# A fused attention and two-MLP kernel: earlier weight rounding, identity transposes at the start, and the gated values' low halves on GpSimd

## The chip, the cores and the metric

The kernel runs on one NeuronCore of a Trainium2 chip. The metric is the device time of one execution in microseconds. The kernel before takes 1164.55 us in the median of 3 runs (1164.22 to 1164.59).

## The reference

Sparse-threshold attention over 4 batches, 8 heads, 576 tokens and a head dimension of 64, then two MLPs over the 2304 tokens (512 to 2048 to 512), all in float32:

```python
scores = scale * q @ k.T
thresh = max(scores, -1) - tau
scores = where(scores >= thresh, scores, -1e9)
attn = softmax(scores)            # sum + 1e-9
x = (attn @ v) as [2304, 512]
h = x @ w_in1;  g = h * sigmoid(1.702 * h);      x = g @ w_out1
h = x @ w_in2;  g = h * tanh(softplus(h));       out = g @ w_out2
```

## The kernel before, in words

**Split precision.** Most products are made of three matmuls on values that are split into a rounded high half and the remainder, the low half: high times low, low times high, high times high. ScalarE writes the high half with a copy to a rounded type (lines with `_hi`), and another engine subtracts it from the raw value to get the low half (`_lo`). The low half lies in the same memory as the raw value. Batch 0's first 16 query tiles (steps 0 to 15) do without the split: their scores, transposes and PV products are plain float32 matmuls.

**Steps.** Attention is cut into N = 144 steps. Each handles one tile of 128 query rows against all 576 keys. All engines run the same software pipeline over a step counter n, each with an order written out by hand. For a step n TensorE makes the scores (`pe_scores`, one step ahead), VectorE takes the row maximum (`dve_max`), GpSimd works out the threshold (`pool_row`), ScalarE takes the exponential (`act_exp`), VectorE masks and sums (`dve_mask`, `dve_inv`, one step later), GpSimd or ScalarE normalises (`pool_norm` for the first 16 steps, `act_norm` afterwards), and two steps later TensorE transposes the probabilities by five matmuls with the identity (`pe_turn`), ScalarE copies them out of PSUM (`act_p_hi`) and VectorE writes their low half (`dve_p_lo`, from step 16 on). After each group of two or three steps TensorE multiplies with v (`pe_pv`), and the result is copied to x. In the first 16 steps this happens at even n: `act_x_first` copies the 64 rows of x from PSUM, and after every second head `act_x_hi_first` rounds a quarter of the first chunk of x, of which `dve_x_lo_first` writes the low half at the next n.

**The first MLP beside attention.** The tokens are taken in 9 chunks of 256 columns. Its work is a list of pieces: "up" pieces (two tiles of hidden features, called a pair) and "down" pieces. Each piece is made of two halves of twelve matmuls. `HALVES_AT[n]` says which halves TensorE makes in step n; a table of `READY` steps says from when a chunk's x is there, and the halves are spread evenly between those steps. The first 108 pieces run beside attention; the others (`ALONE`) follow when attention is over. After an up piece ScalarE takes tanh (`act_tanh`), VectorE multiplies (`dve_gate`), ScalarE rounds (`act_g_hi`) and VectorE subtracts (`dve_g_lo`, last in its step). The first down half of a quarter waits for the low halves of its two pairs.

**The weights of the first MLP** come in 16 pieces of 512 KB, in the order `W_ORDER`. `W_SLOT` gives each the step at which ScalarE rounds it (`act_w_hi`). SyncE issues the load four steps before. The low half is made in two halves, in the same step and the next on GpSimd (`pool_w_lo`), and for the first `W_FIRST` weights one step later on VectorE (`dve_w_lo`).

**Then** the second MLP runs alone, bound by TensorE; the change does not touch it.

A slot list of the tables, as the code works them out before the change: chunk 0 is ready at step 19, chunk 1 at step 43, and the last of 56 pairs beside attention is taken in the last steps. Between the second half of an up pair and the down half that needs it are three steps or more.

Of the kernel before, what the change touches and what calls it, by code (L numbers as in the profile page):

```python
# [29 lines left out]
GROUPS = []  # L30
# [73 lines left out]
for c in range(CHUNKS):  # L104
# [5 lines left out]
    CHUNK_GROUP.append(need)  # L110
READY = [GROUPS[g][4] + (4 if c == 0 else 8) for c, g in enumerate(CHUNK_GROUP)]

# [41 lines left out]
def thresholded_attention_two_mlps(nc, qt, kt, vt, tau, w_in1, w_out1, w_in2, w_out2, out):  # L154
# [3 lines left out]
    with ExitStack() as ctx:  # L158
# [209 lines left out]
        W_ORDER = [0, 1, 2, 3, 8, 9, 4, 5, 10, 11, 6, 7, 12, 13, 14, 15]  # L368
        W_SLOT = dict(zip((9, 12, 14, 17, 19, 21, 23, 24, 26, 28, 30, 31, 33, 34, 36, 37), W_ORDER))

# [8 lines left out]

        W_FIRST = 4  # L380

# [72 lines left out]
        def pe_scores(pe, n):  # L454
# [16 lines left out]
            for half in range(2):  # L471
# [4 lines left out]
                for t, (hd, u, kk) in enumerate(todo):  # L476
                    mm = pe.matmul(ps_s[:, 2 * (n % 2) + half, 0:HS], q_st[u % 2][:, q_cols(hd, i)],  # L477
                                   kk[u % 2][:, cols], start=t == 0, stop=t == len(todo) - 1)
            mm.then_inc(s["qk_done"], 1)

        def pe_turn(pe, n, tiles=range(NJ)):
# [187 lines left out]
        def act_g_hi(act, pair):  # L669
            hi, _, raw = slot_of(pair)  # L670
            act.wait_ge(s["h_read"], pair + 1)
            act.copy(hi, raw).then_inc(s["g_hi_done"], 1)

        def dve_g_lo(dve, pair):
# [214 lines left out]
        def _(pe):  # L889
            pe.wait_ge(s["ident_ready"], 1)  # L890
            pe_scores(pe, 0)
            for n in range(N + 3):
                if n < FRONT + 2:
                    if n >= 2:
                        pe_turn(pe, n - 2)
                    pe_scores(pe, n + 1)
                    if n - 3 in GROUP_AT:
                        pe_pv(pe, GROUP_AT[n - 3])
                    continue
                halves = HALVES_AT[n]  # L900
# [39 lines left out]
        def ups_at(n):  # L940
            return ups(PIECES_AT[n]) if 0 <= n < N + 3 else []

        @block.scalar
        def _(act):
            for n in range(-1, N + 4):
                for pair in ups_at(n - 1):
                    act_tanh(act, pair)
                if n < FRONT + 3:
                    if 0 <= n - 1 and not normed_by_pool(n - 1):
                        act_norm(act, n - 1)  # L950
                    if n >= 0:
                        act_exp(act, n)
                    if n >= 2:
                        act_p_hi(act, n - 2)
                    if n - 3 in GROUP_AT:
                        act_x_first(act, GROUP_AT[n - 3])
                    if n in X_HI_FIRST:
                        act_x_hi_first(act, X_HI_FIRST[n])
                    for u in Q_SCALE.get(n, []):
                        act_q_scale(act, u)  # L960
# [52 lines left out]
        def _(dve):  # L1013
# [3 lines left out]
            for n in range(-1, N + 4):  # L1017
# [17 lines left out]
                if n - 1 in X_HI:  # L1035
                    dve_x_lo(dve, X_HI[n - 1])
                if n - 1 in X_HI_FIRST:
                    dve_x_lo_first(dve, X_HI_FIRST[n - 1])
                if FRONT <= n - 2 < N:
                    dve_p_lo(dve, n - 2)  # L1040
                for pair in ups_at(n - 2):
                    dve_g_lo(dve, pair)
            for pair in ups_at(N + 2):
                dve_g_lo(dve, pair)
            last = []
# [34 lines left out]
        def _(pool):  # L1080
# [3 lines left out]
                               base=0, pattern=[[-1, P]], channel_multiplier=1).then_inc(s["ident_ready"], 1)  # L1084
            for n in range(-1, N):
                if n >= 1 and normed_by_pool(n - 1):
                    pool_norm(pool, n - 1)
                if n >= 0:
                    pool_row(pool, n)
                for u in KQ_PREP.get(n, []):  # L1090
                    pool_k_lo(pool, u)
                for u in V_PREP.get(n, []):
                    pool_v_lo(pool, u)
                for half in range(2):
                    if n - half in W_SLOT and w_place(W_SLOT[n - half]) > W_FIRST:
                        pool_w_lo(pool, W_SLOT[n - half], half)

        def sp_k(sp, u):
# [27 lines left out]
        def _(sp):  # L1126
# [8 lines left out]
            for n in range(N + 4):  # L1135
# [5 lines left out]
                if n - 3 in GROUP_AT:  # L1141
                    g = GROUP_AT[n - 3]
                    u = GROUPS[g][3]
                    if LAST_GROUP[u] == g and u + 2 < len(USES):
                        sp_v(sp, u + 2)
                if n + 4 in W_SLOT:
                    w_load(sp, 0, W_SLOT[n + 4])
                for g in groups_summed(n):
# [69 lines left out]
```

## Time and profile before

| | before |
|---|---|
| median of 3 runs | 1164.55 us |
| the profiled execution, its own time | 1164.05 us |
| its span, first to last instruction | 1162.3 us |
| mean granted TensorE clock | 0.995 |
| attention stage (last transposes of probabilities) | up to 647 us |

In the rows below PE is TensorE's matmul stream, PEld its weight loads, DVE VectorE, ACT ScalarE, POOL GpSimd, SPq SyncE's queue. A row of a timeline gives the start, the duration, the engine, the line of the code, output and inputs and the number of instructions merged; in brackets stands how long the engine had been idle and what released it. A group's row gives its busy time and the mean of one in ns, then the idle time before it.

### The profile page before, as it was taken

What the parts mean: (1) busy time and instruction counts of PE and PEld (TensorE: products, weight loads), DVE (VectorE), ACT (ScalarE), POOL (GpSimd) and SP (SyncE); (2) the same over time, 40 slices, a digit from 0 to 9 for tenths busy, and PEclk for the clock granted to TensorE, in tenths of its full rate; (3) what the DMA queues carried; (4) which work ended last, traced back from release to release, by engine and by line L of the source; (5) the groups of instructions that cost most, each with busy time, mean ns of one, the idle gap of its engine ahead of it and who ended that gap; (6) DMA issues with size and microseconds to landing.
All of it is one profiled execution on the core that took longest, in us unless ns stands there. A gap on an engine that the chain in (4) does not pass through costs nothing.

```text
span 1162.3 us, 19359 instructions
## 1 busy us (share of the span) xinstructions
PE 1118.1 (96%) x7472; PEld 1035.4 (89%) x7472; DVE 759.1 (65%) x1359; ACT 724.1 (62%) x995; POOL 295.4 (25%) x502
## 2 busy tenths in 40 slices
PE   8978889999999999999999999999999999999998
PEld 4568889998999999999999999998999989899997
DVE  4678788888888888888888434665433444344343
ACT  3678787767777777777767322467545554554453
POOL 3557674434444433344333000000000000000000
PEclk9989999999999999999999999999999999999999
DMA  2443534232143222233231003520010000000000
GB/s 65 140 131 114 158 86 111 59 94 85 48 111 91 64 82 77 79 105 83 70 103 28 26 19 106 190 76 28 6 49 1 28 28 28 28 28 28 1 28 27
DMA packets 92923, 78.71 MB, mean 68 GB/s; under 512 B 47520, under 2 KB 78752, under 8 KB 92832
## 3 DMA queue, kind: packets, MB, share of 16 engines
q1 hardware_dynamic: 92832, 77.49, 22.9%
q8 instruction: 59, 0.97, 0.4%
q14 instruction: 32, 0.26, 0.1%
HBM read 63.83 MB, written 13.63 MB: 67 GB/s over the span
## 4 chain that ended last, share of the span: by engine, by line
PE 78%; DVE 11%; ACT 7%; issue 3%; POOL 0%; DMA 0%; SPq 0%; ACTq 0%; DVEq 0%
PE ps_s L743 17%; PE ps_r L628 14%; PE ps_r L648 11%; PE ps_r L766 9%; PE ps_t L492 6%; PE ps_t L513 5%; PE ps_t L766 4%; PE ps_s L477 4%; PE ps_t L648 3%; PE ps_r L513 2%; PE ps_s L466 2%; DVE x_pair L585 2%; DVE pt_lo L574 2%; ACT pv_half_sb L544 1%; DVE neg_max L554 1%
## 5 line engine op out<-in xcount | busy, mean ns | idle before, releaser
L628 PE MATMUL ps_r<-x_hi,wi_lo 128*128 128x256 f32 x544 | 158.5, 291 | 2.7 <-DVE x_lo L701 2.7
L810 DVE COPY hidden<-ps_s 128x768 f32<-128x768 f32 x48 | 45.8, 956 | 170.5 <-PE ps_s L743 170.5
L628 PE MATMUL ps_r<-x_lo,wi_hi 128*128 128x256 f32 x544 | 154.2, 284 | 0.0
L628 PE MATMUL ps_r<-x_hi,wi_hi 128*128 128x256 f32 x544 | 154.2, 283 | 0.0
L492 PE MATMUL ps_t<-ident,e_buf 128*128 128x128 f32 x720 | 118.1, 283 | 27.1 <-DVE pt_lo L574 14.5
L839 ACT ACTIVATE m_lo_raw<-m_lo_raw 128x1536 f32<-128x1536 f32 x24 | 35.8, 1491 | 168.8 <-DVE m_lo_raw L817 168.8
L561 DVE SCALAR_TENSOR_TENSOR e_buf<-ps_s,neg_thr,e_buf 128x576 f32<-128x576 f32 x144 | 117.0, 813 | 29.4 <-ACT e_buf L521 22.9
L648 PE MATMUL ps_r<-g_hi,wo_lo 128*128 128x256 f32 x464 | 135.4, 292 | 0.0
L537 ACT CAST pt_hi<-ps_t 128x640 fp32r<-128x640 f32 x128 | 89.0, 695 | 71.8 <-PE ps_t L492 69.6
L743 PE MATMUL ps_s<-x_hi,wi_lo 128*128 128x384 f32 x384 | 129.0, 336 | 2.4 <-DVE x_lo L799 2.4
L492 PEld LDWEIGHTS ps_t<-ident,e_buf 128*128 128x128 f32 x720 | 84.7, 143 | 52.1 <-issue 29.2
L648 PE MATMUL ps_r<-g_lo,wo_hi 128*128 128x256 f32 x464 | 130.9, 282 | 0.0
L648 PE MATMUL ps_r<-g_hi,wo_hi 128*128 128x256 f32 x464 | 130.9, 282 | 0.0
L743 PE MATMUL ps_s<-x_hi,wi_hi 128*128 128x384 f32 x384 | 128.5, 335 | 0.0
L743 PE MATMUL ps_s<-x_lo,wi_hi 128*128 128x384 f32 x384 | 128.4, 334 | 0.0
L594 POOL TENSOR_SCALAR neg_thr<-neg_max,tau_sb 128x1 f32<-128x1 f32 x144 | 61.7, 428 | 244.2 <-DVE neg_max L554 244.1
L521 ACT ACTIVATE e_buf<-ps_s,neg_max 128x576 f32<-128x576 f32 x144 | 106.4, 739 | 13.5 <-DVE neg_max L554 12.5
L574 DVE TENSOR_TENSOR pt_lo<-ps_t,pt_hi 128x640 fp32r<-128x640 f32 x128 | 104.9, 820 | 14.2 <-ACT pt_hi L537 12.4
L532 ACT ACTIVATE e_buf<-e_buf,even_share,inv_sum 128x576 f32<-128x576 f32 x128 | 111.4, 870 | 3.1 <-DVE inv_sum L569 1.8
L554 DVE TENSOR_REDUCE neg_max<-ps_s 128x1 f32<-128x576 f32 x144 | 107.6, 747 | 8.0 <-PE ps_s L466 7.2
L628 PEld LDWEIGHTS ps_r<-x_hi,wi_lo 128*128 128x128 f32 x544 | 105.7, 194 | 2.9 <-DVE x_lo L701 2.9
L628 PEld LDWEIGHTS ps_r<-x_lo,wi_hi 128*128 128x128 f32 x544 | 104.5, 192 | 0.0
(105 smaller groups left out, 3009.9 us busy)
## 6 DMA issues: line engine op xcount, KB each, us to landing
k_ll_raw<-in_k SPq DMA_DIRECT2D x56, 288.0 KB, 2.9
v_st_raw<-in_v SPq DMA_DIRECT2D x64, 160.0 KB, 2.9
wi_lo_raw<-in_moe_w_in SPq DMA_DIRECT2D x16, 512.0 KB, 3.8
wo_lo_raw<-in_moe_w_out SPq DMA_DIRECT2D x16, 512.0 KB, 4.8
q_raw<-in_q SPq DMA_DIRECT2D x32, 192.0 KB, 2.9
x_scratch<-y_acc SPq DMA_DIRECT2D x9, 512.0 KB, 3.2
x_lo_raw<-x_scratch SPq DMA_DIRECT2D x6, 768.0 KB, 4.7
out_rows<-rows_out SPq DMA_DIRECT2D x18, 256.0 KB, 2.1
```

Source lines behind the costliest of these rows:

```text
L492: mm = pe.transpose(t_flat[:, j * P:(j + 1) * P], e_buf[n % 3][:, j * P:(j + 1) * P], ident[:, :])
L513: mm = pe.matmul(pv_bank(g)[out_rows, 0:w], v[:, j, :], pt[:, j, :], start=j == 0 and part == 0, stop=j == NJ - 1 and part == len(parts) - 1)
L521: act.activation(halves(e_buf[n % 3][:, 0:S]), scores(n), ACT.Exp, bias=neg_max[:, n % 4:n % 4 + 1], scale=-1.0).then_inc(s["exped"], 1)
L532: act.activation(e, e, ACT.Identity, bias=even_share[:, n % 4:n % 4 + 1], scale=inv_sum[:, n % 4:n % 4 + 1]).then_inc(s["normed"], 1)
L537: act.copy(pt_of(n)[0], turned_tile(n)).then_inc(s["p_hi"], 1)
L554: dve.tensor_reduce(neg_max[:, n % 4:n % 4 + 1], scores(n), AX.XY, ALU.min).then_inc(s["maxed"], 1)
L561: dve.scalar_tensor_tensor(out=e, in0=scores(n), scalar=neg_thr[:, c], in1=e, op0=ALU.is_le, op1=ALU.mult, accum_out=row_sum[:, c]).then_i ...
L574: dve.tensor_tensor(lo, turned_tile(n), hi.bitcast(F32), ALU.subtract).then_inc(s["p_lo"], 1)
L628: mm = pe.matmul(bank[:, part * CH:(part + 1) * CH], wi[w][:, k, f * P:(f + 1) * P], x[:, k, :], start=t == 0, stop=t == 3 * KT - 1)
L648: mm = pe.matmul(bank[:, part * CH:(part + 1) * CH], wo[w][:, f, d * P:(d + 1) * P], g[:, at_:at_ + CH], start=t == 0, stop=t == 11)
L743: mm = pe.matmul(ps_s[:, u, 0:CH2], wi[w][:, k, f * P:(f + 1) * P], x[:, k, :], start=t == 0, stop=t == 3 * KT - 1)
L766: mm = pe.matmul(down2_banks[tt], g_[:, fl, tt * P:(tt + 1) * P], wo[w][:, f, :], start=j == 0 and fl == 0 and step == 0, stop=j == NG - 1 ...
```

## The change

Six edits:

- TensorE makes 12 transposes of the identity into an unused part of a PSUM bank before the first scores, and 3 more at the end of each of the steps 0 to 3 (`pe_idle`).
- The weights' slots move to earlier steps, the first from 9 to 4; the low halves of the first seven, not four, are made on VectorE; the loads are issued three steps ahead, not four.
- Chunk 0 counts as ready one step earlier: the first up half is in step 18 and no longer 19, and the halves up to step 36 are spread a little differently. From step 37 on the list is as before.
- For that, the last quarter's low half of x is made on VectorE in step 18, no longer in step 19, and in step 18 ScalarE rounds x before it copies the transposed probabilities, no longer after.
- The low halves of the 56 gated pairs taken beside attention are made on GpSimd, behind the threshold of the step, no longer on VectorE.
- GpSimd's loop therefore runs four steps longer. The 16 pairs after attention stay on VectorE.

```diff
-READY = [GROUPS[g][4] + (4 if c == 0 else 8) for c, g in enumerate(CHUNK_GROUP)]
+READY = [GROUPS[g][4] + (3 if c == 0 else 8) for c, g in enumerate(CHUNK_GROUP)]
...
-        W_SLOT = dict(zip((9, 12, 14, 17, 19, 21, 23, 24, 26, 28, 30, 31, 33, 34, 36, 37), W_ORDER))
+        W_SLOT = dict(zip((4, 6, 8, 10, 12, 14, 16, 18, 21, 23, 26, 28, 30, 31, 34, 35), W_ORDER))
...
-        W_FIRST = 4
+        W_FIRST = 7
...
+        def pe_idle(pe, count):
+
+            for _ in range(count):
+                pe.transpose(ps_r[:, 1, 384:512], ident[:, :], ident[:, :])
...
+        def pool_g_lo(pool, pair):
+            hi, lo, raw = slot_of(pair)
+            pool.wait_ge(s["g_hi_done"], pair + 1)
+            pool.tensor_tensor(lo, raw, hi.bitcast(F32), ALU.subtract).then_inc(s["g_lo_done"], 1)
...
         def _(pe):
             pe.wait_ge(s["ident_ready"], 1)
+            pe_idle(pe, 12)
             pe_scores(pe, 0)
...
                         pe_pv(pe, GROUP_AT[n - 3])
+                    if n < 4:
+                        pe_idle(pe, 3)
                     continue
...
-                    if n >= 2:
+                    if 2 <= n < FRONT + 2:
                         act_p_hi(act, n - 2)
                     if n - 3 in GROUP_AT:
                         act_x_first(act, GROUP_AT[n - 3])
                     if n in X_HI_FIRST:
                         act_x_hi_first(act, X_HI_FIRST[n])
+                    if n == FRONT + 2:
+                        act_p_hi(act, n - 2)
...
-                if n - 1 in X_HI_FIRST:
-                    dve_x_lo_first(dve, X_HI_FIRST[n - 1])
+                for late in (1, 0):
+                    if n - late in X_HI_FIRST and (X_HI_FIRST[n - late] < KT - 1) == (late == 1):
+                        dve_x_lo_first(dve, X_HI_FIRST[n - late])
                 if FRONT <= n - 2 < N:
                     dve_p_lo(dve, n - 2)
-                for pair in ups_at(n - 2):
-                    dve_g_lo(dve, pair)
-            for pair in ups_at(N + 2):
-                dve_g_lo(dve, pair)
...
-            for n in range(-1, N):
+            for n in range(-1, N + 4):
                 if n >= 1 and normed_by_pool(n - 1):
                     pool_norm(pool, n - 1)
-                if n >= 0:
+                if 0 <= n < N:
                     pool_row(pool, n)
+                for pair in ups_at(n - 2):
+                    pool_g_lo(pool, pair)
...
+            for pair in ups_at(N + 2):
+                pool_g_lo(pool, pair)
...
-                if n + 4 in W_SLOT:
-                    w_load(sp, 0, W_SLOT[n + 4])
+                if n + 3 in W_SLOT:
+                    w_load(sp, 0, W_SLOT[n + 3])
```

## Rows read from the trace of the kernel before

**Rows 1.** The page, part 1: busy time, share of the span and instructions of each engine.

```profile
PE 1118.1 (96%) x7472; PEld 1035.4 (89%) x7472; DVE 759.1 (65%) x1359; ACT 724.1 (62%) x995; POOL 295.4 (25%) x502
```

**Rows 2.** Stretches: busy time of PE, PEld, DVE, ACT, POOL; PEclk, DMA share, GB/s.

```profile
70.00:80.00 10.00, 6.12 (x34) 5.00 (x33) 7.82 (x16) 6.64 (x12) 6.15 (x8) 0.81 0.72 230
80.00:90.00 10.00, 9.93 (x70) 9.70 (x69) 6.37 (x13) 7.46 (x13) 5.73 (x9) 0.85 0.16 44
...
650.00:700.00 50.00, 50.00 (x417) 50.00 (x416) 18.42 (x27) 11.25 (x19) 0.00 (x0) 1.00 0.08 24
```

**Rows 3.** Waits of TensorE over the span: us in total, times, longest.

```profile
PE ps_t L492 <- DVE pt_lo L574: 14.5, 27, 1.6
PE ps_t L492 <- DVE x_pair L585: 5.5, 9, 1.0
```

**Rows 4.** Timeline from 0 to 30 us: start, duration, engine, line.

```profile
1.16 0.29 POOL L1083 TENSOR_SCALAR_AFFINE_SELECT ident<-ident 128x128 f32<-128x128 f32 x1 [0.24 <-POOL ident L1081]
...
4.34 4.17 PE L466 MATMUL ps_s<-k_ll_raw,q_raw 64*128 64x288 f32 x8 [4.34 <-ACT q_raw L405]
...
8.27 0.82 DVE L561 SCALAR_TENSOR_TENSOR e_buf<-ps_s,neg_thr,e_buf 128x576 f32<-128x576 f32 x1 [0.81 <-ACT e_buf L521]
...
10.94 0.82 DVE L561 SCALAR_TENSOR_TENSOR e_buf<-ps_s,neg_thr,e_buf 128x576 f32<-128x576 f32 x1 [0.81 <-ACT e_buf L521]
...
14.90 1.33 PE L492 MATMUL ps_t<-ident,e_buf 128*128 128x128 f32 x5
...
16.16 2.28 PE L466 MATMUL ps_s<-k_ll_raw,q_raw 64*128 64x288 f32 x4
...
26.35 1.23 PE L466 MATMUL ps_s<-k_ll_raw,q_raw 64*128 64x288 f32 x4
...
26.80 0.82 DVE L561 SCALAR_TENSOR_TENSOR e_buf<-ps_s,neg_thr,e_buf 128x576 f32<-128x576 f32 x1 [4.09 <-ACT e_buf L521]
...
27.52 0.77 PE L492 MATMUL ps_t<-ident,e_buf 128*128 128x128 f32 x5
```

**Rows 5.** Timeline of the steps from 39 to 54 us.

```profile
39.99 1.04 ACT L365 CAST wi_hi<-wi_lo_raw 128x1024 fp32r<-128x1024 f32 x1
...
50.62 0.36 ACT L550 COPY x_lo_raw<-ps_r 64x256 f32<-64x256 f32 x1 [1.71 <-PE ps_r L513]
...
50.89 1.04 ACT L365 CAST wi_hi<-wi_lo_raw 128x1024 fp32r<-128x1024 f32 x1
...
53.29 0.74 PE L492 MATMUL ps_t<-ident,e_buf 128*128 128x128 f32 x5 [0.85 <-ACT pt_raw L537]
```

**Rows 6.** VectorE's halves of the weights: durations, minimum/median/maximum in ns.

```profile
L385 DVE TENSOR_TENSOR wi_lo<-wi_lo_raw,wi_hi x8: 681/862/1236, 41.1 to 75.9; 128x512 fp32r<-128x512 f32 x8
```

**Rows 7.** Timelines of ScalarE, VectorE and TensorE from 60 to 84 us.

```profile
72.84 0.40 ACT L697 CAST x_hi<-x_lo_raw 128x256 fp32r<-128x256 f32 x1
...
77.06 0.41 DVE L701 TENSOR_TENSOR x_lo<-x_lo_raw,x_hi 128x256 fp32r<-128x256 f32 x1
...
62.14 4.06 PE L513 MATMUL ps_r<-pt_hi_raw,v_st_raw 128*64 128x256 f32 x10
...
77.53 0.58 PE L628 MATMUL ps_r<-x_hi,wi_lo 128*128 128x256 f32 x1 [2.67 <-DVE x_lo L701]
...
80.25 1.27 PE L492 MATMUL ps_t<-ident,e_buf 128*128 128x128 f32 x5
```

**Rows 8.** Groups of instructions, by form: VectorE 190 to 640, GpSimd 83 to 190 us.

```profile
L677 DVE TENSOR_TENSOR g_lo<-g_lo_raw,g_hi 128x512 fp32r<-128x512 f32 x44 | 29.9, 681 | 0.0
...
L390 POOL TENSOR_TENSOR wi_lo<-wi_lo_raw,wi_hi 128x512 fp32r<-128x512 f32 x8 | 10.2, 1292 | 1.6 <-ACT wi_hi L365 1.6
```

**Rows 9.** Waits of GpSimd (190 to 640 us) and of VectorE (83 to 190 us).

```profile
POOL neg_thr L594 <- DVE neg_max L554: 208.9, 95, 5.8
...
DVE e_buf L561 <- POOL neg_thr L594: 2.9, 4, 1.3
```

**Rows 10.** The page, part 6: DMA issues, KB each, us to landing.

```profile
wi_lo_raw<-in_moe_w_in SPq DMA_DIRECT2D x16, 512.0 KB, 3.8
```

## The prediction

> **What bounds the kernel now.** I read the page's busy times first, then a table of stretches, then TensorE's waits, and then the timeline of the first 95 us. TensorE is busy 1118.1 us of 1162.3 [rows 1], so the whole idle time is 44 us and no edit that leaves its 7472 matmuls alone can bring more than that, except by its clock. The stretches show where slack is: behind 650 us TensorE is filled wholly [rows 2], and the change touches nothing there. What the change can move is the idle of the attention stage and the stretches at the lower clock. The waits name two releasers to look at, VectorE's low half of the probabilities (14.5 us in 27 waits) and its sum of the PV halves (5.5 us in 9) [rows 3], and the timeline a third, the first rounding of x, with a single wait of 2.67 us [rows 7].
>
> The clock matters as much. The granted clock column shows 1.00 for the first 60 us, but the same instructions tell another story: four score matmuls take 2.28 us at 16.16 and 1.23 us at 26.35, five transposes 1.33 us at 14.90 and 0.77 us at 27.52 [rows 4]. So TensorE ran at the lower level (1.2 GHz) from its first matmul until about 25 us and at 2.4 GHz from there. The step at 62.14 is low again (ten PV matmuls in 4.06 us), and the column shows two more low parts: 0.81 and 0.85 in 70 to 90 us, which is (0.19 + 0.15) x 10 x 2 = 6.8 us at 1.2 GHz [rows 2, 7].
>
> **The change part by part.** The sum is made against the profiled execution's own 1164.05 us, 0.5 under the median of 1164.55.
>
> *Identity transposes.* The identity is ready at 1.45 us and the first scores start at 4.34, held by the scaling of q [rows 4]. Twelve transposes at the low level start about every 0.21 us (five in 1.33, tail included), so 2.7 us: they fit into this idle time. If they bring the clock up, the first steps run at the pace of the chain on VectorE and ScalarE, which is 10.94 - 8.27 = 2.67 us a step [rows 4]; the two score matmul sets before the first masking take half the time, which brings that masking from 8.27 to about 7.2. Steps 1 to 4 take 2.67. Step 5 has PV before it: two steps hold twice 2.0 us of transposes and scores and about 2.0 of PV (half of the 4.06 in [rows 7]), 6.0 against 5.3 of chain, so 3.3 for it, and a weight's rounding (next part) adds 0.95. These give 7.2 + 10.7 + 4.2 = 22.1 for the masking of step 5, now at 26.80: -4.7 us. Three transposes a step then cost 0.4 us in steps where TensorE has 2.0 us of work in 2.67: hidden. If the clock stays low, the same three cost 0.65 us in steps in which TensorE has no gap, as 14.90 + 1.33 and 16.16 + 2.28 show, for the three steps from 1 to 3: +2.0 us. What the rows say is uneven: turns and scores follow each other without a gap from 14.90 on and did not raise the clock; the PV matmuls behind them did. No row has a run of transposes alone. I take -4.7 and keep +2.0 as the other end.
> The Trainium skill, "TensorE: Matmul & The Clock Gate", Part 4 on the transpose, says that transposes do not count as activity for the clock; by it this part would be +2.0 and the total 6.7 us later. The rows just named fit it, but fit as well that scores with half the rows count little.
>
> *Seven weights, sooner.* A weight's high half on ScalarE takes 1.04 us. At an odd step it is hidden (39.99). At an even step from 4 on it stands between the copy of x, which waits for PV, and the exponential: 50.62, 50.89, and TensorE's next transposes wait 0.85 us at 53.29 [rows 5]. The slots are now 9, 12, 14, 17, then 19 on; they become 4, 6, 8, 10, 12, 14, 16. Slot 4's is in the sum above; of the other six, two stood at even steps already: four more at 0.95 (0.85, and up to 1.04 where x is rounded too) are +3.8 us. Three more weights also bring six more halves to VectorE, 0.86 us each in the median [rows 6], into a gap of 0.81 us before the masking [rows 4]: about 0.15 each, +0.9. Together +4.7, bounds +1 (the wait hides in slack of PV steps) and +7. The loads are issued one step less ahead, three steps instead of four; three steps are at least 8 us, and a load lands in 3.8 us [rows 10], so this costs nothing; without that cover it would be a stall of the landing time at one weight. Behind step 18 three weights fewer are left: 3.1 us less on ScalarE and six halves less on GpSimd.
>
> *x rounded sooner, first up half one step earlier.* Now the last quarter's high part ends at 73.24, but its low part stands in the next step of VectorE, at 77.06, and TensorE waits 2.67 us for it, falls to 1.2 GHz and runs low until 83.0 (the 3.0 low microseconds of the stretch from 80, taken as its start) [rows 2, 7]. After the change a copy that stood ahead of the rounding goes behind it, so x's high part ends at 73.24 at the latest, and the low part (0.41) follows in the same step, at 73.7. The first half (twelve matmuls, 2.72 us low, so 1.4 us at 2.4 GHz) then runs before step 17's transposes, the second behind step 20's scores. With about 1.1 us for those two between them (five transposes 0.77, the split scores less than the 1.23 of the plain ones, overlapped) step 18's transposes come at 73.7 + 1.4 + 1.1 + 1.4 = 77.6 instead of 80.25, 2.6 us sooner and with one half, 1.4 us, more done; and the low clock from 80.25 to 83.0 costs 1.4 less. -5.4 us, bounds -6.4 (the copy's time gained too) and -2.7 (the wait alone). The low stretch at 62.14 (1.7 us lost) I leave as it is: it follows ScalarE's wait in a step that keeps its work.
>
> *The gated low halves.* 56 pairs leave VectorE. Each takes 0.68 us there [rows 8], last in its step, before the next masking; where that masking waited for the exponential anyway the time was hidden. What TensorE can get back is at most its waits on VectorE, 14.5 + 5.5 less 1.5 before 83 us = 18.5 us in 34 waits. A pair falls in about 4 of 10 steps, and one step's waits are cut by at most 0.68: I take -7, bounds 0 and -12. GpSimd gets the same subtraction at its own price, by the weights' halves of the same shape 1.29 us [rows 8], 56 x 1.29 = 72 us. It waits 208.9 us for the row maximum in 95 steps of 190 to 640 us [rows 9], 2.2 us a step, more than one subtraction; and the down projection uses a pair three steps or more after it was taken. But queued behind the subtraction are the low parts of k and v and then the next threshold, for which VectorE's masking waits; between 83 and 190 us that already costs 2.9 us in 4 waits [rows 9]. In 12 of the 56 steps the pair meets k and v both. I take +1.5; bounds 0 and +7 (12 times 0.6).
>
> **Sum.** -4.7 + 4.7 - 5.4 - 7 + 1.5 = -10.9: 1153.1 us, a median some tenths higher.
>
> **The rivals.** *The clock does not rise at the start.* Everything else as above: 1153.1 + 6.7 - 0.95 (slot 4's rounding is then hidden under TensorE's longer step) = 1158.8. For it: the gap-free low stretch from 14.90 on [rows 4]. Against it: that stretch holds only a third of transposes.
> *Only the front counts.* TensorE's small waits are replaced by ScalarE's, since ScalarE feeds the low half's subtraction, and the part of the gated halves nets nothing: 1153.1 + 5.5 = 1158.6.
> *GpSimd becomes late (the other sign).* Its subtraction delays the threshold, the masking and with it the next transposes. At 0.6 us for each of 56 pairs it is +34 in place of -7 + 1.5, 1192; it decides from 0.1 us a pair on (the other three terms come to -5.4, and 56 x 0.1 = 5.6). For it: the 4 waits between 83 and 190. Against it: the 2.2 us of idle a step behind 190.
> *More is gained than VectorE's visible waits*, because steps are bound by the chain of several short gaps that the busy time hides: another 5 to 8 us, about 1146.
>
> **How the numbers follow.** The sum's case has 0.45, the low clock 0.2, the front alone 0.13, the larger gain 0.12, GpSimd late 0.1. The likeliest gives 1153.0, rounded. Leaving out the far half of the larger gain and GpSimd's case, the range is 1145 to 1161.5. A measurement can tell 0.2%, 2.3 us: slower holds GpSimd's case and little more, 0.08; the same takes 0.05 from the low clock and front-only cases together; faster 0.87.
>
> **What would show it.** Right: from the second set of scores on four score matmuls take about 1.2 us and not 2.3, and the masking of step 5 stands near 22; the first up half starts near 73.7 (start and weights cancel), without a wait of microseconds, and the clock column shows no 0.8 in 70 to 90; waits of about 0.9 us for the copy of the probabilities at even steps from 6 to 16; TensorE's waits for the low half fall from 14.5 to about 8; GpSimd's waits for the maximum fall by about 60 us, and VectorE's for the threshold stay under 6. The prediction is wrong if the clock is low in the first 20 us, if the masking waits for the threshold in most pair steps, or if a step in 20 to 43 becomes bound by ScalarE, so that what the front gains is waited away there.

## The result, and the profile after

The changed kernel takes 1166.14 us in the median of 20 runs (1164.86 to 1172.46), the kernel before 1164.32 us (1163.68 to 1165.31, 20 runs). The ratio is 1.0025 with a 95% interval from 1.0017 to 1.0032: a quarter of a per cent slower, where I forecast 1153 in a range from 1145 to 1161.5. The runs also scatter more: ten lie between 1164.9 and 1165.8, seven between 1166.5 and 1168.2, three at 1172; the three have the lowest mean granted clock, 0.982. The profiled execution is one of the ten, 1165.02 us.

The totals hide what happened. TensorE's busy time and the span are nearly what they were [rows 1]; this is the same line of the page of the changed kernel:

```profile
PE 1120.0 (96%) x7496; PEld 1037.3 (89%) x7496; DVE 732.0 (63%) x1309; ACT 723.9 (62%) x995; POOL 351.9 (30%) x552
```

GpSimd has taken 56 us over, VectorE has given 27 us away, and nobody is faster. The start of VectorE's masking, step by step, shows where time went. Differences are against the kernel before, each from one profiled execution:

| masking of step | 2 | 5 | 13 | 18 | 22 | 28 | 43 | 142 | span |
|---|---|---|---|---|---|---|---|---|---|
| before, us | 13.62 | 26.80 | 52.61 | 73.19 | 93.15 | 120.98 | 187.21 | 637.75 | 1162.3 |
| changed, difference | +0.0 | +3.2 | +6.0 | +5.4 | +1.7 | -0.2 | -0.1 | +0.6 | +0.6 |

So 3.2 us are lost up to step 5, another 2.7 up to step 13, 3.7 are won between steps 18 and 22, 1.9 more up to step 28, and between steps 43 and 142 0.7 us are lost again. The four parts follow in this order. (The last column stops at step 142. The masking of step 143 is only 0.1 us later than before, because no subtraction of a gated half stands ahead of it on VectorE any more; TensorE is 0.6 us later there too.)

How far can such a difference be trusted? Two kernels shown further down change nothing that acts before step 17, and their maskings of step 13 still stand 0.2 and 1.0 us later than in the kernel before. A difference of 1 us in one profile may be that of the execution.

**The clock did not rise.** The timeline of the first 31 us of the changed kernel:

```profile
1.50 2.82 PE L484 MATMUL ps_r<-ident 128*128 128x128 f32 x12 [1.50 <-POOL ident L1095]
...
4.35 4.18 PE L466 MATMUL ps_s<-k_ll_raw,q_raw 64*128 64x288 f32 x8
...
13.40 2.29 PE L466 MATMUL ps_s<-k_ll_raw,q_raw 64*128 64x288 f32 x4
...
15.62 0.90 PE L484 MATMUL ps_r<-ident 128*128 128x128 f32 x3
...
16.31 1.27 PE L497 MATMUL ps_t<-ident,e_buf 128*128 128x128 f32 x5
...
17.51 2.29 PE L466 MATMUL ps_s<-k_ll_raw,q_raw 64*128 64x288 f32 x4
...
21.63 2.28 PE L466 MATMUL ps_s<-k_ll_raw,q_raw 64*128 64x288 f32 x4
...
23.84 4.17 PE L518 MATMUL ps_r<-pt_hi_raw,v_st_raw 128*64 128x256 f32 x10
...
27.95 0.77 PE L497 MATMUL ps_t<-ident,e_buf 128*128 128x128 f32 x5
...
30.03 0.82 DVE L566 SCALAR_TENSOR_TENSOR e_buf<-ps_s,neg_thr,e_buf 128x576 f32<-128x576 f32 x1
...
30.72 0.74 PE L497 MATMUL ps_t<-ident,e_buf 128*128 128x128 f32 x5 [0.85 <-ACT pt_raw L542]
```

The twelve transposes fill 1.50 to 4.3 us, 0.23 us each, the low pace. The scores behind them still take 2.29 us for four and the five transposes 1.27, as in [rows 4]; only the PV matmuls at 23.84 bring the pace up, at 27.95 five transposes take 0.77. Meanwhile each group of three identity transposes lengthens a step that had no gap: the score sets start at 13.40, 17.51 and 21.63, 4.1 us apart, where they stood 3.5 apart. The masking of step 5 is at 30.03 and not at 26.80. The clock column cannot show this: it reads 1.00 throughout, as it did in the kernel before up to 60 us.

**A weight at an even step costs what [rows 5] said.** The timeline around 50 us of the changed kernel, where x is rounded too:

```profile
49.23 0.36 ACT L555 COPY x_lo_raw<-ps_r 64x256 f32<-64x256 f32 x1 [1.70 <-PE ps_r L518]
...
49.94 1.04 ACT L365 CAST wi_hi<-wi_lo_raw 128x1024 fp32r<-128x1024 f32 x1
...
52.34 0.74 PE L497 MATMUL ps_t<-ident,e_buf 128*128 128x128 f32 x5 [1.29 <-ACT pt_hi_raw L542]
53.01 1.24 PE L466 MATMUL ps_s<-k_ll_raw,q_raw 64*128 64x288 f32 x4
```

ScalarE copies x, rounds it, rounds the weight, and TensorE's transposes, which need the copy of the probabilities behind them, wait 1.29 us; I had allowed up to 1.04 for such a step. The wait without the rounding of x stands at 30.72 (0.85). The clock stays up behind both: the four scores that follow take 1.24 us.

**The handover of x works.** The next rows are the changed kernel's timeline of the first up half, and its windows for the two stretches of [rows 2]:

```profile
76.83 0.41 ACT L707 CAST x_hi<-x_lo_raw 128x256 fp32r<-128x256 f32 x1
...
77.27 0.43 DVE L711 TENSOR_TENSOR x_lo<-x_lo_raw,x_hi 128x256 fp32r<-128x256 f32 x1 [1.39 <-ACT x_hi L707]
...
77.75 0.39 PE L633 MATMUL ps_r<-x_hi,wi_lo 128*128 128x256 f32 x1
```

```profile
70.00:80.00 10.00, 8.29 (x54) 6.23 (x53) 7.67 (x20) 8.41 (x14) 4.29 (x8) 1.00 0.43 124
80.00:90.00 10.00, 8.65 (x64) 7.82 (x64) 7.94 (x17) 8.64 (x16) 7.62 (x12) 1.00 0.40 128
```

The low part of x follows its rounding at once, the first up half starts at 77.75 without a wait of TensorE's matmul stream, against 77.53 with a wait of 2.67 [rows 7], though all steps ahead of it are 5.4 us late. The clock column has no 0.81 and 0.85 any more. It also has no low stretch between 60 and 70 us, where it read 0.83 before; this one comes and goes between executions of the same instructions (0.83 before, 1.00 in the kernel with the gated halves alone, which acts later), and the 0.5 us won between steps 13 and 18 need not be the change's.

**The gated low halves moved a gap and gained nothing.** The four views that follow are of the changed kernel: TensorE's waits over the span, VectorE's waits from 190 to 640 us, GpSimd's waits there, and the group of the moved subtraction there, as in the costliest groups:

```profile
PE ps_t L497 <- DVE pt_lo L579: 14.5, 27, 1.7
PE ps_t L497 <- DVE x_pair L590: 7.5, 12, 2.0
```

```profile
DVE x_pair L590 <- ACT pv_half_sb L549: 36.4, 41, 1.9
DVE e_buf L566 <- ACT e_buf L526: 23.6, 35, 1.1
```

```profile
POOL neg_thr L599 <- DVE neg_max L559: 177.0, 90, 5.8
```

```profile
L682 POOL TENSOR_TENSOR g_lo<-g_lo_raw,g_hi 128x512 fp32r<-128x512 f32 x44 | 56.9, 1293 | 0.0
```

and the same two rows of VectorE's waits from 190 to 640 us in the kernel before:

```profile
DVE x_pair L585 <- ACT pv_half_sb L544: 33.0, 40, 1.9
...
DVE e_buf L561 <- ACT e_buf L521: 7.9, 20, 0.6
```

and, in the changed kernel alone, the waits of TensorE's weight loads for GpSimd's subtraction over the span:

```profile
PEld ps_r L653 <- POOL g_lo L682: 0.6, 2, 0.3
```

TensorE's waits for the low half are 14.5 us in 27 waits in both kernels; those for the sum of the PV halves rose from 5.5 to 7.5 [rows 3]. VectorE's masking now waits 23.6 us for the exponential instead of 7.9. Most of what was taken off VectorE went into such gaps. GpSimd does the subtraction in 1.29 us and waits 177.0 us for the maximum instead of 208.9 [rows 9], 32 us less where I had expected about 60. Twice it is late: the down half's weight loads wait for its result, and the two waits stand at 290 and 454 us, where the maskings fall 0.4 and 0.3 us further behind. Eleven of the profiled kernels of this document have the subtraction on GpSimd, and in all of them the maskings fall back by 0.5 to 0.7 us between steps 43 and 142; in the seven others with a change it is 0.1 to 0.2.

### The profile page after: what moved, and what is told of

Its sections match the earlier page's. It is cut to its first block, busy times and chain, and to the rows that moved or that the text cites. A ratio compares the mean times of both kernels' runs of the same rounds, so it can differ in the third digit from the quotient of the medians.

```text
span 1162.9 us, 19407 instructions
## 1 busy us (share of the span) xinstructions
PE 1120.0 (96%) x7496; PEld 1037.3 (89%) x7496; DVE 732.0 (63%) x1309; ACT 723.9 (62%) x995; POOL 351.9 (30%) x552
## 4 chain that ended last, share of the span: by engine, by line
PE 77%; DVE 10%; ACT 7%; issue 4%; POOL 2%; ACTq 0%; POOLq 0%; DVEq 0%
PE ps_s L753 17%; PE ps_r L633 13%; PE ps_r L653 11%; PE ps_r L776 9%; PE ps_t L497 5%; PE ps_t L518 5%; PE ps_t L776 4%; PE ps_s L477 4%; PE ps_t L653 3%; DVE pt_lo L579 2%; DVE x_pair L590 1%; PE ps_s L466 1%; DVE neg_max L559 1%; ACT pv_half_sb L549 1%; PE ps_r L518 1%
## 5 line engine op out<-in xcount | busy, mean ns | idle before, releaser
L497 PE MATMUL ps_t<-ident,e_buf 128*128 128x128 f32 x720 | 117.3, 282 | 31.9 <-DVE pt_lo L579 14.5
L526 ACT ACTIVATE e_buf<-ps_s,neg_max 128x576 f32<-128x576 f32 x144 | 106.4, 739 | 14.5 <-DVE neg_max L559 13.7
```

The lines of the kernel that those rows point to most:

```text
L497: mm = pe.transpose(t_flat[:, j * P:(j + 1) * P], e_buf[n % 3][:, j * P:(j + 1) * P], ident[:, :])
L526: act.activation(halves(e_buf[n % 3][:, 0:S]), scores(n), ACT.Exp, bias=neg_max[:, n % 4:n % 4 + 1], scale=-1.0).then_inc(s["exped"], 1)
```

## The experiments

Each kernel ran beside the kernel before on the same chip. Times are medians; the masking times beside them are of one profiled execution each, which need not be a typical one.

### Undoing one part of the change

Without the identity transposes:

```diff
-            pe_idle(pe, 12)
...
-                    if n < 4:
-                        pe_idle(pe, 3)
```

> The changed kernel without the 24 identity transposes. Theory A (they only lengthen low-clock steps, and the delay is carried to the end): maskings of steps 5 to 16 come 3 us sooner than in the changed kernel, and the end is 3 us sooner, 1163 us, with the spread of the runs back under 2 us. Theory B (whatever the first 20 steps win or lose is waited away by step 40): the same 3 us at step 5, nothing at step 40 and at the end, 1165 to 1166 us. If the transposes do raise the clock and something else slows the first steps, the masking of step 5 comes later, not sooner.

With the weights as before:

```diff
-        W_SLOT = dict(zip((4, 6, 8, 10, 12, 14, 16, 18, 21, 23, 26, 28, 30, 31, 34, 35), W_ORDER))
+        W_SLOT = dict(zip((9, 12, 14, 17, 19, 21, 23, 24, 26, 28, 30, 31, 33, 34, 36, 37), W_ORDER))
-        W_FIRST = 7
+        W_FIRST = 4
-                if n + 3 in W_SLOT:
-                    w_load(sp, 0, W_SLOT[n + 3])
+                if n + 4 in W_SLOT:
+                    w_load(sp, 0, W_SLOT[n + 4])
```

> The changed kernel with the weights' slots, their split over engines and the loads' lead as before. Theory A: the even slots cost what the steps 6 to 12 show, so the masking of step 12 comes about 3 us sooner than in the changed kernel; between 20 and 43 some of it is given back, since three more weights are rounded there; end 1 to 3 us sooner. Theory B: the end stays within 0.5 us of the changed kernel's.

With the gated low halves on VectorE:

```diff
+                for pair in ups_at(n - 2):
+                    dve_g_lo(dve, pair)
+            for pair in ups_at(N + 2):
+                dve_g_lo(dve, pair)
...
-            for n in range(-1, N + 4):
+            for n in range(-1, N):
...
-                for pair in ups_at(n - 2):
-                    pool_g_lo(pool, pair)
...
-            for pair in ups_at(N + 2):
-                pool_g_lo(pool, pair)
```

> The changed kernel with the gated pairs' low halves on VectorE again. If the low halves on GpSimd bring nothing (VectorE's gain goes into waiting for the exponential), every step from 43 on takes what it takes in the changed kernel and the end is within 0.5 us. If GpSimd's lateness had eaten a real gain, the steps 18 to 43 differ and the end moves by 1 us or more; if VectorE was a bound, this one is 3 us or more slower.

With x's last quarter and the first up half in their old steps:

```diff
-READY = [GROUPS[g][4] + (3 if c == 0 else 8) for c, g in enumerate(CHUNK_GROUP)]
+READY = [GROUPS[g][4] + (4 if c == 0 else 8) for c, g in enumerate(CHUNK_GROUP)]
...
-                    if 2 <= n < FRONT + 2:
+                    if n >= 2:
                         act_p_hi(act, n - 2)
...
-                    if n == FRONT + 2:
-                        act_p_hi(act, n - 2)
...
-                for late in (1, 0):
-                    if n - late in X_HI_FIRST and (X_HI_FIRST[n - late] < KT - 1) == (late == 1):
-                        dve_x_lo_first(dve, X_HI_FIRST[n - late])
+                if n - 1 in X_HI_FIRST:
+                    dve_x_lo_first(dve, X_HI_FIRST[n - 1])
```

> The changed kernel with x's last quarter and the first up half one step later, as before. Theory A: the gain of steps 17 to 22, about 3.7 us in the changed kernel, is gone, TensorE waits 2.7 us and falls to the lower clock near 80 us, and the end is 3 to 5 us later, 1169 to 1171. Theory B: step 40 and the end within 0.5 us of the changed kernel's.

| kernel | median us (runs) | ratio to before, 95% interval | masking against before, step 5 | 13 | 22 | 43 | 142 |
|---|---|---|---|---|---|---|---|
| changed | 1166.14 (20) | 1.0025 (1.0017 to 1.0032) | +3.2 | +6.0 | +1.7 | -0.1 | +0.6 |
| no identity transposes | 1164.51 (11) | 1.0016 (1.0006 to 1.0026) | +1.3 | +4.0 | -0.2 | -2.0 | -1.3 |
| weights back | 1163.18 (12) | 0.9981 (0.9968 to 0.9994) | +2.1 | +2.1 | -1.7 | -1.2 | -0.6 |
| gated halves back | 1166.35 (12) | 1.0014 (1.0006 to 1.0023) | +3.1 | +5.9 | +3.1 | +2.0 | +2.2 |
| x back | 1168.59 (5) | 1.0037 (1.0025 to 1.0049) | +3.3 | +6.0 | +4.5 | +2.8 | +3.5 |

Theory B does not hold: what stands at step 43 is still there at step 142 in every row, within the 0.7 us of the gated halves. Only of the weights' cost is a large part gone by then. The identity transposes cost 1.6 us in the median and 1.9 in the profiles; the spread did not shrink as expected (1163.2 to 1169.9), so they are not its cause. The weights cost 3.0 us in the median: without their shift the rest of the change beats the kernel before. In the profiles they cost 3.8 by step 13, and 2.7 of that come back by step 43; three weights fewer are rounded there, which may be the reason. Undoing x costs 2.5 us, less than the 3 to 5 that were expected.

Undoing the gated halves costs 2.1 us at step 43 in one profile and 0.2 in the medians. Of the 2.1, 1.4 stand already at step 17, before the first pair's subtraction, and this execution has a low stretch of the clock there (0.92 and 0.91 between 60 and 80 us) that the changed kernel's has not. So most of it belongs to the execution and not to the edit.

Two of the twelve runs with the weights back took 1156.0 and 1156.1, and one with the gated halves back 1160.6: some executions are 6 or 7 us faster than the others of the same kernel. That is about what a clock that is up from the start is worth in such a kernel, 5.9 us by the run with plain matmuls and the weights back (1157.33) below; in these executions twelve transposes may have been enough. None of them was traced.

### The kind of instruction that lifts the clock, and where the weights stand

The next three have plain matmuls in place of the identity transposes:

```diff
-                pe.transpose(ps_r[:, 1, 384:512], ident[:, :], ident[:, :])
+                pe.matmul(ps_r[:, 1, 384:512], ident[:, :], ident[:, :], start=True, stop=True)
```

once in the changed kernel,

> The changed kernel with plain 128-row float32 matmuls of the identity in place of its 24 identity transposes, same count and places. Theory A (transposes are what fails to raise the clock; full matmuls raise it): four score matmuls take about 1.2 us from step 1 or 2 on, the masking of step 5 comes at about 22 to 24 us instead of 30.0, and since the front is carried to the end, 6 to 8 us less, 1158 to 1160. Theory B (24 small instructions are too little whatever they are): as the changed kernel, 1166.

once with the other parts of the change undone as above (the kernel before with the 24 matmuls and nothing else),

> The kernel before with only the 24 plain matmuls of the identity added. Theory A: masking of step 5 at about 22 instead of 26.8, end 4 to 5 us sooner, about 1159.5. Theory B: 2 us slower, 1166.

and once with only the weights put back.

> The changed kernel with plain matmuls of the identity and with the weights' slots as before; x sooner and the low halves on GpSimd stay. Theory A: the weights' shift costs 3 us and the low clock 7, so 1155 to 1157, faster than both kernels. Theory B: 1163, as with the weights put back alone.

The fourth moves the first eight weights:

```diff
-        W_SLOT = dict(zip((4, 6, 8, 10, 12, 14, 16, 18, 21, 23, 26, 28, 30, 31, 34, 35), W_ORDER))
+        W_SLOT = dict(zip((5, 7, 9, 11, 13, 15, 17, 19, 21, 23, 26, 28, 30, 31, 34, 35), W_ORDER))
```

> The changed kernel with its first eight weights at steps 5, 7, 9, 11, 13, 15, 17 and 19, one step later each. Theory A (a rounding at an even step from 4 on delays TensorE's transposes by 0.85 to 1.04 us, at an odd step it is hidden): steps 5 to 12 take 3 to 4 us less, some of it carried to the end, 1163 to 1165. Theory C (it is the three additional weights in front of step 18, wherever they stand): within 1 us of 1166.

| kernel | median us (runs) | ratio to before, 95% interval | step 5 | 13 | 22 | 43 | 142 |
|---|---|---|---|---|---|---|---|
| changed, plain matmuls | 1164.13 (11) | 1.0001 (0.9993 to 1.0010) | -2.6 | +3.4 | -0.8 | -2.6 | -2.0 |
| plain matmuls alone | 1159.80 (5) | 0.9962 (0.9950 to 0.9975) | -3.3 | -3.3 | -4.1 | -4.1 | -4.0 |
| plain matmuls, weights back | 1157.33 (5) | 0.9942 (0.9930 to 0.9954) | -3.3 | -3.3 | -7.5 | -6.9 | -6.3 |
| changed, odd slots | 1160.08 (6) | 0.9956 (0.9939 to 0.9972) | +2.4 | +1.5 | -2.9 | -4.7 | -4.0 |

The clock at the start is worth 4.4 us by itself. The odd slots are worth 6 us in the median, more than the 1 to 3 that were expected, and 4.5 by step 13, so my price for an even slot was right in kind: it is the place, not the number, that costs. (Each of these weights is also rounded one step later; that is not separated.) In the odd-slot kernel the same rounding stands here, between two steps' copies, and TensorE's PV follows without a wait (its timeline at 42 us):

```profile
41.54 0.68 ACT L542 COPY pt_raw<-ps_t 128x640 f32<-128x640 f32 x1
...
42.39 0.77 PE L497 MATMUL ps_t<-ident,e_buf 128*128 128x128 f32 x5
...
42.43 1.04 ACT L365 CAST wi_hi<-wi_lo_raw 128x1024 fp32r<-128x1024 f32 x1
...
44.25 2.37 PE L518 MATMUL ps_r<-pt_raw,v_st_raw 128*64 128x256 f32 x10
```

With plain matmuls in the changed kernel I expected 1158 to 1160 and got 1164.1. Its timeline of TensorE and its windows of two microseconds say why:

```profile
22.80 1.23 PE L466 MATMUL ps_s<-k_ll_raw,q_raw 64*128 64x288 f32 x4
24.89 0.74 PE L497 MATMUL ps_t<-ident,e_buf 128*128 128x128 f32 x5 [0.85 <-ACT pt_raw L542]
25.55 1.76 PE L466 MATMUL ps_s<-k_ll_raw,q_raw 64*128 64x288 f32 x4
```

```profile
24.00:26.00 2.00, 1.15 (x8) 0.92 (x8) 1.93 (x7) 1.06 (x3) 0.48 (x1) 1.00 1.06 324
26.00:28.00 2.00, 2.00 (x6) 0.94 (x5) 1.70 (x5) 1.32 (x2) 1.33 (x3) 0.53 0.02 5
```

The even slot's wait of 0.85 us comes when the clock is already up, and behind it the four scores take 1.76 us instead of 1.23 and the column falls to 0.53. From step 5 to step 13 this execution loses 6.0 us against the kernel before, where the changed kernel loses 2.7. Two low stretches, 0.83 in 20 to 30 us and 0.83 in 50 to 60 us, account for the other 3.3: 0.17 x 10 = 1.7 us each. The even slots did not always bring the clock down: behind the same wait, and behind the one of 1.29 us, it stayed up in the changed kernel (30.72 and 52.34 above). And the stretch at 50 to 60 us is also there with odd slots (0.87 with plain matmuls, 0.83 with the larger number of transposes, both below). So this fall behind an even slot was seen once; how often it comes, and whether the wait alone decides it, is open.

### How much it takes

Three kernels on the kernel before, with 60 calls ahead of the first scores and none later, as transposes, as matmuls of the first 64 rows (`ident[0:64, :]` for both operands), and as matmuls of all rows:

```diff
+            pe_idle(pe, 60)
             pe_scores(pe, 0)
```

> The kernel before with 60 identity transposes ahead of the first scores and none later. Theory A (transposes do not raise the clock): all sixty at the low pace, 0.21 us from one to the next, 12.8 us in all, and the first four score matmuls behind them still take about 2.3 us. Theory D (the twelve were too few, and the 64-row scores are what does not count): the pace halves to about 0.11 us inside the sixty. Its end is of no interest: the first scores are pushed back by up to 10 us.

> As the last one, with 60 plain matmuls of the identity's first 64 rows. If half the rows do not raise the clock, all sixty run at the low pace; if they do, the pace halves inside. The kernel before has such scores from 4.3 to 8.5 us without a rise, so the low pace is expected.

> As the last two, with 60 plain matmuls of all 128 rows. Expected by every theory that holds for the PV matmuls at 22 to 25 us: the pace halves within the sixty. If it does not, something other than the kind of instruction decides.

The sixty transposes: timeline of TensorE and windows.

```profile
1.51 9.56 PE L484 MATMUL ps_r<-ident 128*128 128x128 f32 x60 [1.51 <-POOL ident L1094]
11.00 2.20 PE L466 MATMUL ps_s<-k_ll_raw,q_raw 64*128 64x288 f32 x8
14.88 2.25 PE L466 MATMUL ps_s<-k_ll_raw,q_raw 64*128 64x288 f32 x4 [1.68 <-DVE e_buf L566]
```

```profile
1.50:4.50 3.00, 2.99 (x14) 2.99 (x15) 0.00 (x0) 0.91 (x2) 0.00 (x0) 1.00 0.46 120
...
7.50:10.50 3.00, 3.00 (x30) 3.00 (x29) 0.00 (x0) 0.00 (x0) 0.00 (x0) 1.00 0.00 0
...
13.50:16.50 3.00, 1.62 (x4) 1.16 (x4) 1.80 (x5) 1.07 (x3) 1.49 (x5) 0.60 0.25 71
16.50:20.00 3.50, 3.50 (x11) 2.09 (x9) 2.53 (x6) 1.68 (x4) 1.61 (x4) 0.50 0.00 0
```

The sixty with 64 rows, and the sixty with 128 rows (a plain float32 matmul is two instructions in the trace, a transpose is one, hence x120):

```profile
1.50 25.97 PE L484 MATMUL ps_r<-ident 64*128 64x128 f32 x120 [1.50 <-POOL ident L1094]
```

```profile
1.50 15.54 PE L484 MATMUL ps_r<-ident 128*128 128x128 f32 x120 [1.50 <-POOL ident L1094]
16.98 2.21 PE L466 MATMUL ps_s<-k_ll_raw,q_raw 64*128 64x288 f32 x8
20.86 1.21 PE L466 MATMUL ps_s<-k_ll_raw,q_raw 64*128 64x288 f32 x4 [1.68 <-DVE e_buf L566]
...
23.45 2.28 PE L466 MATMUL ps_s<-k_ll_raw,q_raw 64*128 64x288 f32 x4 [0.43 <-DVE e_buf L566]
```

Each of the three ran once. Theory D is right. Sixty transposes take 9.56 us and not 12.8: 14 start in the 3 us up to 4.5 and 30 in the 3 us from 7.5 on. Transposes do raise the clock. The 64-row matmuls run 26 us without a gap and never do: 0.22 us each to the end. So it is likely the scores, with their 64 rows, that do not bring the clock up in the first steps; they have 288 columns where this filler has 128, and were not tried by themselves. With no filler behind the sixty the rise does not last either: in the first kernel TensorE waits 1.68 us at 14.88, the column falls to 0.60 and 0.50, and the scores are slow. In the third, behind the same wait, four scores still take 1.21 us and only those at 23.45 are slow (2.28). What was wrong with the twelve was their number.

Twelve plain matmuls take the time of 24 transposes. The next kernel decides whether that is all:

```diff
-            pe_idle(pe, 12)
+            pe_idle(pe, 24)
...
-                        pe_idle(pe, 3)
+                        pe_idle(pe, 6)
```

with the weights back, to stand beside the 1157.33 above.

> As the run with plain matmuls and the weights as before (1157.3), but with 24 transposes at the start and 6 behind each of the steps 0 to 3 in place of 12 and 3 plain matmuls, the same time on TensorE. Theory amount: the clock rises before the first scores, masking of step 5 at 23.5, 1157 to 1158. Theory kind (a transpose counts less than a matmul): low clock in most runs, masking of step 5 at 28 or later, 1163 or more, with wide spread.

It took 1156.82 us (5 runs, 1156.60 to 1157.60), ratio 0.9940 (0.9928 to 0.9953). TensorE's timeline:

```profile
1.51 4.67 PE L484 MATMUL ps_r<-ident 128*128 128x128 f32 x24 [1.51 <-POOL ident L1095]
6.11 2.20 PE L466 MATMUL ps_s<-k_ll_raw,q_raw 64*128 64x288 f32 x8
...
9.99 1.21 PE L466 MATMUL ps_s<-k_ll_raw,q_raw 64*128 64x288 f32 x4 [0.88 <-DVE e_buf L566]
```

Eight score matmuls in 2.20 us behind 24 transposes, and step 5's masking at 23.02. It was the amount.

### The two remaining parts by themselves, and the version these runs point to

The gated low halves on GpSimd as the only change, and x's last quarter and the first up half sooner as the only change:

> The kernel before with nothing changed but the gated low halves of the attention stage on GpSimd. Theory gain in the few steps with weights: steps 22 to 40 take 1 to 3 us less, later steps the same, 1162 to 1163. Theory nothing: 1164.2 within 0.5. If GpSimd's threshold is late: over 1165.

> The kernel before with nothing changed but x's last quarter rounded and subtracted in step 18 and the first up half in step 18. My prediction had -5.4 us for it (1159); undoing it in the changed kernel cost 2.5 us, so 1161 to 1162 if that carries over.

The first took 1164.81 us (11 runs), ratio 1.0006 (0.9997 to 1.0015): no difference that can be told. Its masking of step 22 stands where it stood, that of step 43 is 0.1 us later and that of step 142 0.6, with the same two waits of the weight loads. Its profile has the same waits of VectorE from 190 to 640 us as the changed kernel's (36.4 and 23.6), so they come from this part. The second took 1161.83 us (11 runs), ratio 0.9982 (0.9973 to 0.9991), and its windows have a clock of 1.00 from 60 to 90 us.

Three combinations:

> The changed kernel with plain matmuls of the identity and the first eight weights at odd steps, 5 to 19. If both repairs add (the clock about -3 to -6 us, the odd slots -6 us), masking of step 12 near 46 and an end at 1153 to 1156, below the 1157.3 of the weights as before. If three more weights in the front cost something by themselves, 1157 to 1159.

> The changed kernel with 24 and 6 identity transposes and the first eight weights at odd steps 5 to 19. As the version with plain matmuls (1155.6), 1155 to 1156.

> The same with the gated low halves on VectorE again. If GpSimd's part is worth what the steps 17 to 40 showed, 1157 to 1158; if it is worth nothing, within 0.5 us of the other one; if it costs, as alone on the kernel before (+0.7), 1154.5 to 1155.

| kernel (5 runs each) | median us | ratio to before, 95% interval | step 5 | 13 | 22 | 43 |
|---|---|---|---|---|---|---|
| plain matmuls, odd slots | 1155.57 | 0.9929 (0.9917 to 0.9942) | -3.3 | -4.2 | -7.8 | -8.4 |
| 24 and 6 transposes, odd slots | 1155.32 | 0.9926 (0.9913 to 0.9938) | -4.2 | -5.1 | -9.3 | -10.0 |
| the same, gated halves on VectorE | 1154.81 | 0.9925 (0.9912 to 0.9939) | -4.0 | -4.9 | -8.5 | -8.6 |

The last two are 9 us below the kernel before. They differ in the gated halves alone and their medians lie 0.5 us apart, the one without the moved halves the lower, with intervals that overlap nearly wholly: that part gains nothing here either. (In the two profiles it looks the other way round, 1.3 us for the moved halves at step 43. That is within what one execution differs from another.)

## Why the prediction was wrong, by its own steps

**Identity transposes: -4.7 forecast, +3.2 at step 5.** This is the first of the two steps that failed, "if they bring the clock up": twelve did not. The other is the gain of the gated halves, below. The mechanism behind it, that a full clock lets the first steps run at the pace of VectorE's chain, was right and nearly of the right size: -4.2 at step 5 with 24 transposes, 4.4 us at the end with plain matmuls alone. What I did not ask was whether twelve are enough. I had the row that spoke against it, gap-free transposes and scores from 14.90 on without a rise, gave that rival 0.2, and took the favourable end of a cost that I had bounded at both. The price of a clock that stays low was also short: +2.0 for this part and 0 for the weight in slot 4, hidden under a longer step. The transposes cost 1.9 by the run without them, and slot 4 cost 1.3: the clock rises in the PV matmuls of that step, before its rounding comes, and TensorE's wait at 30.72 is at the full pace. The sum of the rival with a low clock has a slip as well: the -4.7 that it takes out holds slot 4's 0.95 already, so its terms give 1153.1 + 6.7 = 1159.8 and not 1158.8. The rule of the Trainium skill that I set beside it, that transposes do not count for the clock ("TensorE: Matmul & The Clock Gate", Part 4), gave the right sign here, but the measurement goes against it: in the run with sixty transposes in a row the pace of the same instruction doubles, 14 starts in 3 us and then 30.

**Weights sooner: +4.7 forecast.** +2.7 between steps 5 and 13, 3.8 at step 13 by the run with the weights back (slot 4 included), 3.0 us at the end by the medians and 1.2 by the two profiles. The even-slot wait has the size of [rows 5]. Right as a mechanism; what I did not price is that by step 43 2.7 us come back, and that behind such a wait the clock can fall, as it did once in the kernel with plain matmuls.

**x sooner: -5.4 forecast, -3.7 between steps 18 and 22, 2.2 and 2.5 us at the end.** The wait and the low stretch are gone as said. Too much, as I read it, was the 1.4 us for one half more done: that half is counted out again when the lists meet at step 37, and in between TensorE has idle time anyway. No run isolates this.

**Gated halves: -7 + 1.5 forecast, no gain and some 0.6 us of cost measured.** This is the second step that failed, and it weighs 6 us, nearly as much as the first. Alone, the part gives a ratio of 1.0006 (0.9997 to 1.0015). The cost side was near: GpSimd takes 1.29 us each, VectorE's masking does not wait more for the threshold (4.7 us over the span, 4.8 before), and what it costs came by another way, the two waits of TensorE's weight loads for GpSimd's result, 0.6 us. The gain did not exist. I took -7 of TensorE's 18.5 us of waits for VectorE as what a shorter VectorE step gives back; those waits went from 14.5 + 5.5 to 14.5 + 7.5. But VectorE is late with the low half in those steps because it waits itself, for ScalarE's copy of the PV half (33.0 us of such waits from 190 to 640 us in the kernel before, the first of the two rows of it shown above and not among my rows; 36.4 in the changed one), and what the removed subtraction sets free lies ahead of the masking, which then waits for the exponential. That the freed time goes into these waits is shown by the run with this part alone; that they are why TensorE's waits did not shrink is what the rows suggest, and no run tests it.

**The sum.** I had given the low clock 0.2 at 1158.8, and "only the front counts" 0.13. What came is both at once: I had treated them as alternatives, and by their own terms the two together give 1153.1 + 6.7 + 5.5 = 1165.3. In the profile the parts are +3.2 + 2.7 - 0.5 - 3.7 - 1.9 + 0.1 + 0.7 = +0.6 at step 142. That the median lies 1.8 us above the kernel before, while the profiled execution ends 0.6 us later, comes from the scatter of the changed kernel's runs. Its cause is open. That the clock falls at the even slots, as in the run with plain matmuls, would fit the three runs at 1172 with their mean clock of 0.982; it does not fit the others, of which those with 0.989 took 1165.2 to 1165.8 us and those with 0.997 took 1166.5 to 1168.2.

## What to carry to other kernels

Before pricing a warm-up, read from the trace what the instructions behind it do to the clock: here 64-row matmuls did not raise it, and twelve fillers were too few where 24 were enough. Place an extra operation by what waits behind it in its queue, not by how early it can be: one step's difference was worth 6 us. Give the same change more than one execution before you read 1 us out of a profile. And subtract nothing for work taken off an engine until the trace shows that the engine, and not its own wait, is what the next one waits for.

## What the runs showed of the hardware that was not expected

- The clock column read 1.00 at the start of every profile, whatever the level. In the kernel with 60 transposes it shows 1.00 in the stretch in which 14 start in 3 us and in the one in which 30 do. At the start of these kernels the level had to be read from durations.
- Gap-free 64-row float32 matmuls left TensorE at 1.2 GHz for 26 us. 128-row matmuls and transposes of 128 rows brought it to 2.4 GHz in the same place (one run of each).
- Some executions of one kernel end 6 to 7 us before the others (1156.0 beside 1163.2, 1153.4 beside 1160.1), about what the clock's rise at the start is worth. All kernels that showed it have twelve transposes. The kernels with the larger filler and the first eight weights at odd steps did not show it in 15 runs (1154.4 to 1157.4), nor did the kernel before in any of its runs (1163.4 to 1165.5).
